# First transfer in halves, first chunk closed at once, first dense unit reordered: a retention-plus-two-MLP kernel

## The reference

```python
state = gamma * state + k[t] (outer) v[t]          # 8 heads of 64, gamma = 1 - 2**(-5 - h)
y[t]  = scale * q[t] @ state                       # decayed linear attention, per batch and head
x = y as [1536, 512]
h = x @ w_in                                       # 512 -> 2048
x = (h * sigmoid(1.702 * h)) @ w_out               # 2048 -> 512
xn = x / sqrt(mean(x*x) + 1e-6) * rms_g
g = xn @ w_gate; val = xn @ w_val                  # 512 -> 1536 each
out = (g * sigmoid(g) * val) @ w_out2              # 1536 -> 512
```

## Time and profile before

| | us |
|---|---|
| median of 3 runs | 584.25 (584.05 to 584.41) |
| the profiled execution | 583.44 |
| its span, first to last instruction | 581.6 |
| PE busy in it | 573.3 (99%) |
| DVE / ACT / POOL busy | 359.2 / 298.1 / 172.1 |

### The profile page before, as it was taken

How to read it: one execution, slowest core, us unless ns; L and a number is a source line. 1 busy time by engine, 2 the same in 40 slices (tenths; PEclk the granted TensorE clock), 3 DMA queues, 4 the chain that set the end, 5 groups by cost and what they waited for, 6 DMA issues and landing times.

```text
span 581.6 us, 9400 instructions
## 1 busy us (share of the span) xinstructions
PE 573.3 (99%) x3640; PEld 551.8 (95%) x3640; DVE 359.2 (62%) x486; ACT 298.1 (51%) x501; POOL 172.1 (30%) x222
## 2 busy tenths in 40 slices
PE   7999999999999999999999999999999999999997
PEld 7988999999999999999999999998889999998886
DVE  5797555676425667775346768678755666666432
ACT  1244766645336766645237655574444555564321
POOL 2386444000222452000314464410051545420000
PEclk9999999999999999999999999999999999999999
DMA  8981222322112222312202222233213322224202
GB/s 319 392 292 37 74 72 73 108 73 73 38 36 73 72 74 70 111 39 72 73 0 74 73 74 72 74 84 99 73 36 125 93 73 73 73 74 112 69 1 108
DMA packets 24220, 52.84 MB, mean 91 GB/s; under 512 B 1776, under 2 KB 1904, under 8 KB 24176
## 3 DMA queue, kind: packets, MB, share of 16 engines
q1 hardware_dynamic: 23600, 50.41, 28.2%
q10 hardware_dynamic: 576, 1.84, 0.8%
HBM read 49.09 MB, written 3.15 MB: 90 GB/s over the span
## 4 chain that ended last, share of the span: by engine, by line
PE 97%; DVE 1%; DMA 1%; issue 0%; ACT 0%
PE bank L539 20%; PE twin L539 20%; PE twin L480 11%; PE twin L483 11%; PE twin L482 11%; PE bank L483 6%; PE bank L480 6%; PE bank L482 6%; PE twin L392 2%; PE bank L438 2%; PE bank L425 1%; DMA arena<-attn_in 1%; PE bank L409 1%; DVE x_lo L787 0%; PE bank L580 0%
## 5 line engine op out<-in xcount | busy, mean ns | idle before, releaser
L778 DVE TENSOR_TENSOR w_lo<-raw,w_hi 128x512 fp32r<-128x512 f32 (+2 forms) x148 | 149.3, 1024 | 49.7 <-ACT w_hi L612 49.5
L1059 POOL TENSOR_TENSOR raw<-raw 128x256 f32<-128x256 f32 x40 | 32.1, 803 | 317.1 <-DMA raw<-w 312.5
L480 PE MATMUL twin<-x_hi,w_hi 128*128 128x384 f32 x360 | 120.5, 335 | 0.6 <-ACT arena L676 0.6
L483 PE MATMUL twin<-x_hi,w_lo 128*128 128x384 f32 x360 | 120.3, 334 | 0.0
L482 PE MATMUL twin<-x_lo,w_hi 128*128 128x384 f32 x360 | 120.2, 334 | 0.0
L612 ACT ACTIVATE w_hi<-raw 128x512 fp32r<-128x512 f32 (+2 forms) x148 | 109.0, 763 | 18.0 <-PE bank L539 7.6
L813 DVE TENSOR_TENSOR g_lo<-arena,g_hi 128x768 fp32r<-128x768 f32 x56 | 54.3, 970 | 74.8 <-ACT g_hi L642 74.8
L642 ACT ACTIVATE g_hi<-arena 128x768 fp32r<-128x768 f32 x56 | 47.5, 848 | 103.6 <-PE bank L539 103.6
L480 PEld LDWEIGHTS twin<-x_hi,w_hi 128*128 128x128 f32 x360 | 67.6, 188 | 0.9 <-ACT arena L676 0.9
L482 PEld LDWEIGHTS twin<-x_lo,w_hi 128*128 128x128 f32 x360 | 67.6, 188 | 0.0
L483 PEld LDWEIGHTS twin<-x_hi,w_lo 128*128 128x128 f32 x360 | 67.6, 188 | 0.0
(11 more groups left out here) (105 smaller groups left out, 995.9 us busy)
## 6 DMA issues: line engine op xcount, KB each, us to landing
raw<-w SPq DMA_DIRECT2D x68, 512.0 KB, 3.7
arena<-attn_in SPq DMA_DIRECT2D x22, 512.0 KB, 7.9
out<-x SPq DMA_DIRECT2D x1, 1536.0 KB, 8.6
out<-x SPq DMA_DIRECT2D x6, 256.0 KB, 2.0
arena<-attn_in ACTq DMA_DIRECT2D x2, 512.0 KB, 10.1
arena<-tables ACTq DMA_DIRECT2D x1, 512.0 KB, 6.1
arena<-tables ACTq DMA_DIRECT2D x1, 256.0 KB, 9.8
ident<-ident_in SPq DMA_DIRECT2D x1, 64.0 KB, 12.8
```

Of the source, the lines that this page charges most:

```text
L480: pe.matmul(dst, w_hi[q][:, w], x_hi[:, x], start=start and kk == 0, stop=False, skip_group_check=True)
L483: mm = pe.matmul(dst, w_lo[q][:, w], x_hi[:, x], start=False, stop=kk == 1, skip_group_check=True)
L778: dve.tensor_tensor(w_lo[q % 3][:, dst], src, w_hi[q % 3][:, dst].bitcast(F32), ALU.subtract)\
L1059: pool.tensor_tensor(s1, a21, a22, ALU.add).then_inc(w_sums, 1)
```

## The change

The first half of chunk 0 now comes in two transfers, queries by SP's queue and keys by ACT's, each 256 KB, at the head of either queue. The values of chunk 0 move from ACT's queue to SP's second place, those of chunk 1 from SP's to ACT's, those of chunk 2 from ACT's to SP's. The mask moves from ACT's first place to its second. `qk_at` and `kv_at` give the counts to wait for (slot 0 counts 32 for its first use). `from_chunk` waits for `kv_in` in every chunk. `load_kv(4)` also waits for `kv_done`. On PE, 12 fill matmuls instead of 3 follow the first scores, and then chunk 0 is finished before the scores of chunk 1. On DVE the first `new_state` goes before the first `decay_q`.

In the first dense unit, PE runs product 6 ahead of product 3; DVE runs both remaining sums of x first, then `lower_x` of T2 and T3, and `lower_w` last; ACT runs `split_x(0, T4)` behind `copy_u2` instead of ahead of the weight piece of unit 1.

```diff
-FILL = 3
+FILL = 12
-LOWER = {True: (B11, B21, T1, B22, T3, T2, T4), False: (B11, B21, T1, T2, B22, T3, T4)}
+LOWER = {True: (B11, B21, T1, B22, T2, T3, T4), False: (B11, B21, T1, T2, B22, T3, T4)}
@@ sync
+        def qk_at(a):
+            return 16 * (a // SLOTS) + (32 if a % SLOTS == 0 else 16)
+        def kv_at(a):
+            return 16 * (a // SLOTS) + 16
-            load(0)
+            sp.dma_start(slot[0][:, 0:512], attn_in[0, :, 0:512]).then_inc(qk_in[0], 16)
+            load_kv(0)
             load(1)
-            load_kv(1)
+            load_kv(2)
             load(2)
             load(3)
             load_kv(3)
...
+                    if b == SLOTS:
+                        sp.wait_ge(kv_done, 1)
                     load_kv(b)
@@ tensor
-                if a % CHUNKS == CHUNKS - 1:
-                    pe.wait_ge(kv_in[a % SLOTS], 16 * (a // SLOTS) + 16)
+                pe.wait_ge(kv_in[a % SLOTS], kv_at(a))
...
                 scores(a)
                 if a == 0:
-                    for _ in range(FILL):
-                        pe.matmul(gate[1][:, 0:P], ones[:, :], ones[:, :], start=True, stop=True)
+                    fill(FILL)
+                    from_state(0)
+                    from_chunk(0)
+                    new_products(0)
                 scores(a + 1)
                 if a == 0:
-                    new_products(0)
-                    from_state(0)
-                    from_chunk(0)
                     from_state(1)
                     new_products(1)
...
                     pe.wait_ge(w_lo_done, lo_at[r] + 2)
+                    product(6, n, 2, 1, 2, T2, False)
                     pe.wait_ge(m5_copied, n + 1)
                     product(3, n, 1, 1, 3, B22, False)
-                    product(6, n, 2, 1, 2, T2, False)
@@ scalar
+            act.dma_start(slot[0][:, 512:1024], attn_in[0, :, 512:1024]).then_inc(qk_in[0], 16)
             act.dma_start(mask, tables[:, T_MASK:T_Q]).then_inc(mask_in, 16)
-            act.dma_start(slot[0][:, 1024:2048], attn_in[0, :, 1024:2048]).then_inc(kv_in[0], 16)
             act.dma_start(q_table, tables[:, T_Q:T_ALL]).then_inc(q_table_in, 16)
-            act.dma_start(slot[2][:, 1024:2048], attn_in[2 * BATCH, :, 1024:2048]).then_inc(kv_in[2], 16)
+            act.dma_start(slot[1][:, 1024:2048], attn_in[BATCH, :, 1024:2048]).then_inc(kv_in[1], 16)
...
+                    split_next(r, 0)
+                    copy_u2(n)
                     if n == 0:
                         split_x(0, T4)
-                    split_next(r, 0)
-                    copy_u2(n)
@@ vector
                 if a == 0:
+                    new_state(0)
                     decay_q(1)
-                    new_state(0)
...
                 if a == 10:
                     sum_x(0, T2)
+                    sum_x(0, T4)
+                    lower_x(0, T2)
+                    lower_x(0, T3)
                     lower_w(0, 2)
-                    lower_x(0, T3)
-                    lower_x(0, T2)
...
                     else:
-                        sum_x(0, T4)
                         lower_x(0, T4)
```

More of the change, by code:

```diff
@@ L385, in scores @@
                 q, k = slot[r][:, 0:512], slot[r][:, 512:1024]
-                pe.wait_ge(qk_in[r], 16 * (a // SLOTS) + 16)
+                pe.wait_ge(qk_in[r], qk_at(a))
                 if a >= 2:
@@ L402, in new_products @@
                 v = slot[r][:, 1536:2048]
-                pe.wait_ge(kv_in[r], 16 * (a // SLOTS) + 16)
+                pe.wait_ge(kv_in[r], kv_at(a))
                 pe.wait_ge(k_decayed, m + 1)
@@ L444, in _, with fill @@
             pe.wait_ge(ones_set, 1)
-            for _ in range(WARM_UP):
-                pe.matmul(gate[1][:, 0:P], ones[:, :], ones[:, :], start=True, stop=True)
+            def fill(count):
+                for _ in range(count):
+                    pe.matmul(gate[1][:, 0:P], ones[:, :], ones[:, :], start=True, stop=True)
+            fill(WARM_UP)
             for a in range(0, STEPS, 2):
@@ L918, in decay_q @@
                     dve.wait_ge(q_table_in, 16)
-                dve.wait_ge(qk_in[r], 16 * (a // SLOTS) + 16)
+                dve.wait_ge(qk_in[r], qk_at(a))
                 if x >= 2:
@@ L1039, in decay_k @@
                 r, m = a % SLOTS, state_at(a)
-                pool.wait_ge(kv_in[r], 16 * (a // SLOTS) + 16)
+                pool.wait_ge(kv_in[r], kv_at(a))
                 if m >= 2:
@@ L1048, in decay_q @@
                 r, x = a % SLOTS, cross_at(a)
-                pool.wait_ge(qk_in[r], 16 * (a // SLOTS) + 16)
+                pool.wait_ge(qk_in[r], qk_at(a))
                 if x >= 2:
```

## The result

The changed kernel took 586.27 us (median of 13 runs, 584.87 to 589.0), the kernel before beside it 584.31 us (13 runs, 583.52 to 585.33): ratio 1.0044, 95% interval 1.0034 to 1.0054. Timed twice more beside other kernels it came to 585.51 (12 runs, ratio 1.0023, 1.0012 to 1.0034) and 585.50 us (10 runs, ratio 1.0025, 1.0013 to 1.0038). The profiled execution took 584.87 us with a span of 583.1, 1.4 and 1.5 us more than before. In the first comparison the medians lie 1.96 us apart and the means 2.6. So the changed kernel is slower, by 0.2 to 0.4%, and its times are spread over 4 us where those of the kernel before are spread over 2. That spread is the part of the story that the prediction lacks.

What follows compares the result with a forecast made beforehand. PE, busy 573.3 us or 99% of the span, was taken as the bound, with the attention stage also held by transfers. Attention 0 and dense unit +1.18 on 584.25 gave 585.4 us (+0.20%), range 584.2 to 586.7.

Steps and rivals of the forecast that it cites:

- The first transfer: Start: the halved first pair saves 1.3 us, so scores start at 5.4 us; the mask lands 1.2 us later, at 8.1.
- The fills: Start: 12 fills end at 12.4 us (10.6 to 13.8), so chunk 2's scores start at 18.4 instead of 17.03.
- rival of the overrun: Start: fills at half pace push chunk 2's scores past 18.34 us; 586.2 us in the middle, up to 586.9; chance 0.13.
- The attention stage: Held by PE's work and transfers; slack of 1.31 us takes nearly all the lateness: 0 taken, -0.3 to +1.5 us.
- carried lead: Attention stage: 1.3 us of earlier start come through, plus 0.84 with no new dense wait: 582.1 us; chance 0.08.
- halves without effect: Start: first pair still lands at 6.7 us, everything from the mask on 1.3 us later: 586.7 us; chance 0.07.
- The dense unit: First dense unit: 0.84 us stall before product 7 gone, but unit 1 late behind its weight piece: +1.18 us net.
- rival of the short weight piece: Before unit 1: POOL pauses while DVE lowers the weight piece, so net only +0.65 us, 584.9 us; chance 0.20.
- no new wait: First dense unit: reordering takes the 0.84 us away and nothing is late: 583.4 us; chance 0.10.
- The sum: Whole kernel: attention 0 and dense unit +1.18 us give 585.4 us, +0.20%; chance 0.42.
- simply follows PE: Whole kernel: PE is busy 99% of the span, and everything behind the first stages was taken to follow it.
- within 0.2%: Whole kernel: outcome within 0.2% of the kernel before, given chance 0.47, against 0.45 slower and 0.08 faster.

Runs made afterwards that it cites:

- e1: The changed kernel again with no edit: 585.51 us, ratio 1.0023.
- e3: The kernel before with only the change of the start, dense unit as before: 584.56 us (11 runs), ratio 1.0009.
- e4: The changed kernel with ACT's split of T4 moved back ahead of the weight piece of unit 1: 583.84 us (12 runs), ratio 0.9995.
- e5: The changed kernel with 5 matmuls on ones put into PE's wait before unit 1: 586.03 us (5 runs), ratio 1.0031.
- e6: The changed kernel with ACT's split of T4 later still, behind the activation and second weight piece: 587.96 us (6 runs), ratio 1.0056.
- e9: e6 with 9 matmuls on ones put into PE's wait before unit 1: 586.55 us (5 runs), ratio 1.0040.
- e7: The kernel before with product 6 ahead of product 3 and DVE's new order, ACT's order untouched: 583.45 us (11 runs), ratio 0.9986.
- e12: The changed kernel unchanged, run again for a trace: 587.44 us with a mean clock of 0.997.
- e13: The changed kernel unchanged, run again for a trace: one run, 585.22 us, clock 1.000.
- e14: The kernel before, unchanged, run for a trace: 584.32 us with a mean clock of 0.997.
- e2: The kernel before with only the change of the first dense unit: 585.04 us (11 runs), ratio 1.0021.

## Where the prediction was right, and why it missed the time

- **The first transfer.** Forecast scores at 5.4, mask at 8.1, `masked(0)` done by 9.6; measured 5.52, 8.31 and 9.67. The pairwise sharing of the two queues, by which it was worked out, fits.
- **The fills.** Forecast to end at 12.4 (10.6 to 13.8), measured 11.2; full pace came back sooner than the 5.6 us that I carried over. In the traces it came back at quite different moments: the 24 fill rows took 3.79 us here, 3.63 in e1, 2.94 in e3 and e4. Chunk 2's scores started at 17.37, inside the slack, which ended at 18.34, so the rival of the overrun is out. Even in e5 and e6, with fills of 4.26 and 4.34 us, they started at 17.62 and 17.72.
- **The attention stage.** Forecast 0. Its end, the extra matmul of unit 0, came at 50.41, 51.30, 51.16, 50.50 and 51.50 in five traces with the old start, and at 50.79, 50.51, 50.86, 50.33, 51.29, 50.76, 50.81 and 50.97 in eight with the new one in which the clock did not fall ahead of it (e5, e6 and e9 gave 51.62, 51.73 and 50.51). No difference between old and new start can be seen (means 50.97 and, with e5, e6 and e9, 50.93), whether chunk 2 started at 16.1 or 17.5. The rivals of the carried lead and of the halves without effect are out.
- **The dense unit.** Forecast +1.18 us net: the stall of 0.84 gone, and a weight piece of 1.49 us that starts late. Measured 8.32 - 7.38 + 0.10 = +1.04 in the profiled execution, the piece again 1.49 us beside POOL's sums. The lowering of T4 ahead of it took 0.96, and the wait 1.63 where about 1.8 was forecast. In the other traces of the changed kernel the distance was 8.34, 8.34, 8.33, 8.65 and 8.80. The rival of the short weight piece is out, and so is "no new wait" for this kernel; it is what e7 does, at the 0.84 us worked out for it.
- **What failed.** The sum had +1.18 us; the medians of the first comparison lie 1.96 us apart and its means 2.6. The step that failed is the one that turns the new stall into a price: PE, ready at 57.05, starts unit 1 at 58.86, the unit is late by 1.18 us, and what comes behind "simply follows PE". That took the wait for the whole price and put at nothing, without a reason, what happens to PE's pace behind an idle stretch; no rival named it either. The runs showed a second term in its place: in 10 of 36 runs of the changed kernel the mean clock was 0.997 or less, and these took 586.1 to 589.0 us (median 588.0), the other 26 a median of 585.48 (with e12 and e13 it is 11 of 38). The undisturbed ones lie 1.19 us above the kernel before (584.29, 73 runs), which meets the forecast to the hundredth by luck; the 10 lie 2.4 us higher in the mean and add 10/36 x 2.4 = 0.7 us to it. Six of the 13 runs of the first comparison were of this kind, which brought its median to +2.0; the seven others have a median of 585.92, 0.4 us above that of all 26, so not all of the miss in that comparison is the clock. In the one dear execution that was traced, the loss is accounted for: e12 took 2.22 us more than e13, of which about 1.6 are the slow matmuls, 0.53 an attention stage that ended at 51.29 instead of 50.76, and 0.15 the longer way from unit 0 to unit 1. What the other nine lost, no trace shows. So 586.27 lies within the range given, but 0.9 us above the forecast, and the chance given to "within 0.2%" was too high.

What is shown: the place of the fall in e12 and e6, behind the wait, and in e14, at the start. That idle time of PE is its cause is not shown beyond that: it rests on e6 against e9 (4 of 6 against 0 of 5) and on e3 (0 of 11); e5 did not support it, and e4, without the wait, had 2 of 12. Open is why such a wait lets the clock fall in one execution in four and not in the others. Its length alone doesn't decide: the clock fell behind 1.78 us of idle PE in e4 and held behind 2.00 in e3, 1.94 in e13 and 1.93 in e2. The Trainium skill ("TensorE: Matmul & The Clock Gate", section "Part 1: The HAM clock gate") describes a gate with two states, set by recent activity and looked at on a schedule of its own that does not start with the kernel. The two levels agree with the traces (1.00 and 0.50 and nothing between in the clock records of all 17; the windows show averages over both); a schedule of its own would fit the changing moment of the rise, but no run here shows the schedule itself.

## What to carry to other kernels

When a reordering takes a stall away, follow each moved step to whoever stands behind it on its own engine: here ACT's split of T4 was moved behind a copy that waits for PE, and the first weight piece of the next unit stood behind T4 on DVE. A new idle stretch of TensorE of 1.6 to 2.1 us in the middle of a dense stage can have two prices, itself and a share of executions in which the clock falls (here 10 in 36, at 2.4 us, the place of the fall shown in one trace); look at the spread and at each run's mean clock, not at one trace. And where a stage is held by its transfers, as here, an earlier first chunk or more warm-up changed nothing but where PE waits, and in one trace (e4) the clock fell behind the wait of an early PE.

## What was not expected of the hardware

- The clock fell to half for some 3.4 us (in e12 from 60.4 to 63.8) behind idle stretches of PE of 1.78 us (e4), 2.08 us (e12) and 2.69 us (e6). It held behind 1.63 us (four traces of the changed kernel), 1.93 (e2), 1.94 (e13), 2.00 (e3) and 1.73 (e7, attention stage), and in every trace behind the 0.58 us in the dense stage of the kernel before.
- The mean clock that is printed for an execution doesn't tell the cost: 0.997 in the kernel before cost nothing (e14), in the changed kernel 1.6 us (e12), and the slow pace ahead of the first rise is not in it at all (1.00 in the earlier trace rows).
